# A ring of four PSUM banks for the first eight steps of the last layer, and products nobody reads in TensorE's wait before it

## The reference

```python
x = _attn_ref(q, k, v)                      # 2 x 8 heads, 576 tokens, top 32 scores kept
x = _moe_ref(x, w_gate, w1, w2, capacity)   # 1152 tokens, 8 experts of 288 slots, relu
# the last layer, 1152 tokens, 512 -> 2048 -> 512
h = x @ w_in
h2 = h * h
h3 = h2 * h
P = a[0] + a[1] * h + a[2] * h2 + a[3] * h3
Q = 1.0 + np.abs(b[0]) * np.abs(h) + np.abs(b[1]) * h2
g = P / (Q + 1e-06)
return (g @ w_out).astype(np.float32)
```

## Time and profile before

| | |
|---|---|
| median of 3 runs | 807.46 us |
| lowest, highest | 806.16, 808.84 us |
| the profiled execution | 809.16 us |
| its span (first to last instruction) | 807.4 us |
| mean granted TensorE clock over the span | 0.958 |

### The profile page before, as it was taken

The page is one execution under the profiler, slowest core; times in us unless marked ns, Lnnn a source line. Parts: engine busy times, 40 slices in busy tenths (PEclk is TensorE's granted clock), DMA queues, the critical chain, the costliest instruction groups (busy, mean ns, idle before and its releaser), DMA issues.

```text
span 807.4 us, 15534 instructions
## 1 busy us (share of the span) xinstructions
PE 740.2 (92%) x5370; PEld 692.8 (86%) x5370; DVE 658.3 (82%) x1664; ACT 491.8 (61%) x890; POOL 359.7 (45%) x531
## 2 busy tenths in 40 slices
PE   4899999999999999838999999999469999999997
PEld 4788899898898888728999999999469899898996
DVE  3999999999999999825767667675749988898885
ACT  6677676666677775434445444544547767767673
POOL 4646565545568784240000000000149678667764
PEclk9799999999999999967999999999769999999999
DMA  9640000600000202031657677586811002000001
GB/s 190 159 163 14 1 16 1 222 15 2 14 2 15 106 7 100 1 144 44 219 173 237 194 207 238 170 210 190 230 48 31 1 1 80 1 0 19 22 1 39
DMA packets 61978, 71.20 MB, mean 88 GB/s; under 512 B 21969, under 2 KB 41937, under 8 KB 61906
## 3 DMA queue, kind: packets, MB, share of 16 engines
q1 hardware_dynamic: 60466, 65.57, 27.5%
q0 software_dynamic: 1440, 4.72, 1.7%
HBM read 56.12 MB, written 14.16 MB: 87 GB/s over the span
## 4 chain that ended last, share of the span: by engine, by line
PE 58%; DVE 26%; DMA 5%; issue 4%; ACT 3%; POOL 2%; SPq 1%; DVEq 0%; ACTq 0%; POOLq 0%
PE bank L1400 16%; PE bank L1401 16%; PE bank L1402 16%; DVE best L739 8%; DVE pairs L741 5%; DVE best L760 3%; PE bank L1306 3%; DVE pairs L758 2%; PE bank L1282 2%; PE bank L1272 2%; DMA slots_out<-y_blocks 2%; DVE pairs L722 2%; DMA slot_rows<-slots_in 2%; DVE joined L769 1%; DVE least_kept L778 1%
## 5 line engine op out<-in xcount | busy, mean ns | idle before, releaser
L957 DVE RECIPROCAL r<-c 128x384 f32<-128x384 f32 x48 | 122.5, 2552 | 25.3 <-POOL c L678 25.2
L739 DVE MAX8 best<-pairs 128x8 f32<-128x288 f32 x288 | 130.9, 547 | 0.0
L1028 ACT ACTIVATE probsT<-bank 96x768 f32<-96x768 f32 x72 | 58.2, 808 | 95.5 <-PE bank L1289 95.5
L667 POOL DMA_INDIRECT x_rows<-slots_out,slot_index x9 | 11.2, 1240 | 225.8 <-DMA slots_out<-y_blocks 224.3
L1306 PE MATMUL bank<-v_rows,probsT 96*128 96x65 f32 (+1 forms) x960 | 106.5, 264 | 3.6 <-ACT probsT L1028 3.4
L741 DVE MATCH_REPLACE8 pairs<-best,pairs 128x288 f32<-128x288 f32 x216 | 109.7, 547 | 0.0
L1306 PEld LDWEIGHTS bank<-v_rows,probsT 96*128 96x128 f32 (+1 forms) x960 | 102.3, 181 | 8.0 <-ACT probsT L1028 6.8
L886 DVE TENSOR_TENSOR wl<-raw,wh 128x1024 fp32r<-128x1024 f32 x72 | 87.2, 1218 | 19.6 <-ACT wh L1122 19.2
L1136 ACT ACTIVATE hTh<-bank 128x288 fp32r<-128x288 f32 x64 | 26.5, 414 | 104.4 <-PE bank L1402 104.4
L1400 PE MATMUL bank<-xTh,wh 128*128 128x288 f32 x256 | 76.7, 300 | 12.9 <-DVE xTl L898 12.9
L577 POOL TENSOR_TENSOR pairs<-scores 128x288 int32<-128x288 int32 x72 | 57.7, 801 | 66.3 <-ACT scores L1014 65.9
(11 more groups left out here) (138 smaller groups left out, 2201.6 us busy)
## 6 DMA issues: line engine op xcount, KB each, us to landing
raw<-in_moe_w SPq DMA_DIRECT2D x16, 2048.0 KB, 8.9
slots_in<-zeros SPq DMA_DIRECT2D x18, 256.0 KB
slot_rows<-slots_in SPq DMA_DIRECT2D x32, 144.0 KB, 8.7
slots_out<-y_blocks SPq DMA_DIRECT2D x32, 144.0 KB, 8.2
raw<-in_moe_w_in SPq DMA_DIRECT2D x8, 512.0 KB, 8.0
v_rows<-in_v SPq DMA_DIRECT2D x16, 144.0 KB, 4.0
out_rows<-out_rows SPq DMA_DIRECT2D x9, 256.0 KB, 2.4
q_rows<-in_q SPq DMA_DIRECT2D x8, 256.0 KB, 3.1
```

Source lines behind the costliest of these rows:

```text
L739: ins = nc.vector.max(best, cur)
L957: nc.vector.reciprocal(rS[x][:], cS[x][:]).then_inc(s_d2, 1)
L1028: nc.scalar.activation(pT[x % 2][:], T_ps[0:KP, 0:KJ * P], ACT.Exp, scale=SCALE).then_inc(s_ex, 1)
```

## The change

It has three parts.

1. PE issues 38 matmuls of 128x512 into bank 0 after the last expert product, from weights that are ready by then, and three more after each of the three tiles' transposes. Nobody reads what they write: `in_step(0)` starts bank 0 afresh.
2. The first eight steps' hidden values lie in banks 0, 1, 2, 6, 0, 1, 2, 7 in place of 0, 1, 2, 0, 1, 2, 0, 1. Steps 3 and 7 wait for no g, steps 4 to 6 wait for g of steps 0 to 2 (four steps back), steps 8 to 10 for g of steps 4 to 6, and from step 11 on all is as before, three steps back.
3. Since banks 6 and 7 are lent to steps 3 and 7, the transposes for the next group come after steps 10 to 13, for both groups that have them, on PE, ACT and DVE alike.

```diff
-        T_AT = (8, 9, 10, 11)
+        T_AT = (10, 11, 12, 13)
+        H2_FIRST = (0, 1, 2, 6, 0, 1, 2, 7)
+        def h2_bank(m):
+            return bank(H2_FIRST[m] if m < len(H2_FIRST) else (m - len(H2_FIRST)) % 3)
+        def h2_steps_before(m):
+            return 0 if m in (0, 1, 2, 3, 7) else m - 3 if m < 11 else m - 2
...
-                hp = bank(m % 3)[:, 0:GN]
+                hp = h2_bank(m)[:, 0:GN]
...
+            def keep_busy(times, to, by):
+                for _ in range(times):
+                    nc.tensor.matmul(to, by[:, 0:P], by[:, 0:to.shape[1]], start=True, stop=True)
...
             w2_step(E - 1, 1, FC - 1)
             pe.wait_ge(s_yt, E * DC)
+            pe.wait_ge(s_wl, 4 * (2 * E - 1))
+            keep_busy(38, bank(0), wh[0])
...
                         if i == TG - 1:
                             last.then_inc(s_tb[t_use(d)[0]], 1)
+                    keep_busy(3, bank(0), wh[0])
...
             def in_step(m):
                 g, f = divmod(m, FC2)
-                if m >= 3:
-                    pe.wait_ge(s_g, m - 2)
+                if h2_steps_before(m):
+                    pe.wait_ge(s_g, h2_steps_before(m))
...
-                    last = product(bank(m % 3)[:, 0:GN], wh[sl][:, c:c + P], wl[sl][:, c:c + P],
+                    last = product(h2_bank(m)[:, 0:GN], wh[sl][:, c:c + P], wl[sl][:, c:c + P],
```

## The result

| | before | changed |
|---|---|---|
| median of 4 timed runs, us | 808.04 | 801.75 |
| lowest, highest, us | 806.16, 808.84 | 801.33, 802.91 |
| profiled execution, us (its span) | 809.16 (807.4) | 802.91 (801.2) |
| mean granted TensorE clock | 0.958 | 0.972 |

The ratio is 0.9929 with a 95% interval from 0.9912 to 0.9947, so 5.7 us faster (4.3 to 7.1); the two medians lie 6.3 us apart. It was forecast as 4.6 us, with a median of 802.9.

The account below looks back on a forecast made before the run. PE was taken as the bound from out(0) on, so an earlier out(0) counts in full: 5.2 us less 0.3 gives 4.9, 4.6 against the median, forecasting 802.9 us, range 800.9 to 805.8.

Parts of the forecast that it names:

- step 0: Step after the gathers: held by the tokens' low parts, it lets step 1 start at 595.3, not 596.54; 1.25 us.
- steps 1 and 2: Next two steps on PE: their first matmuls, low before, now run at the high clock; 0.35 us gained.
- the wait: PE's 2.21 us wait for g before step 3 shrinks to 0.3 us before step 4; 1.9 us gained.
- steps 3 and 4: The two steps ahead of out(0): at the high clock 4.18 us in place of 5.90; 1.7 us gained.
- The ties at out(1) and out(2): PE gets to these two outs about when gl(1) and gl(2) end; 0.3 us charged.
- Part 1, the fillers: Gather wait and tiles: 38 matmuls, 10 low, end at 587.6; clock back before step 0 is half done.
- Rival (b): The clock isn't held over the gathers, so step 0 runs low; 3.8 to 2.1 us gained, 804.6; chance 0.16.
- Part 2, the ring: Steps 0 to 3 run without a wait, step 4 waits 0.3 us; out(0) at 604.0, 5.2 us earlier.
- Part 3, the turns: The same eight turns of three transposes, two steps later: nothing added, 3 us of cover left before step 16.
- (c): DVE's chain sets the pace, gl late at steps 5 and 6 and their outs; 2 to 3 us gained, 805.2; chance 0.09.
- (d): The wait at step 4 grows and the clock falls there; 1 to 2 us gained, 806; chance 0.05.
- (e): Slower: fillers run low throughout, end at 593.4, and step 0 starts 8 us later; 811; chance 0.04.

Follow-up runs that it names:

- Ring alone: The changed kernel without any of the 47 filler matmuls; 31.26 us to out(0) against 35.20 before, timed gain 4.3 us (2.8 to 5.7).
- fillers alone: The kernel before plus the 47 filler matmuls, banks and transposes as before; 33.52 us to out(0), timed gain 1.2 us (0.3 to 2.1).
- 60 fillers: The changed kernel with 60 matmuls in the wait in place of 38; 33.68 us to out(0), timed gain 3.2 us (2.1 to 4.4).
- turns alone: The kernel before with only the next group's transposes moved to steps 10 to 13; 35.30 us to out(0), ratio 0.9992 (0.9977 to 1.0006).
- one lent bank: The changed kernel with bank 6 lent to step 3 only, bank 7 taken back; 29.88 us to out(0), timed gain 1.5 us (0.5 to 2.5).

## Why the prediction was right

**The measure.** PE is the bound from out(0) on and the change only shifts it: right, 193.73 and 193.74 us.

**The size.** 5.2 us to out(0) less 0.3 for late gl was forecast, 5.14 measured. By terms: step 0 gave 1.37 (forecast 1.25), steps 1 and 2 0.37 (0.35), the wait 1.93 (1.9), steps 3 and 4 1.47 (1.7), since they took 4.43 us without the wait where I had 4.18. The ties at out(1) and out(2) cost nothing: gl(1) ended at 606.95 and out(1) started at 607.09, gl(2) at 611.12 and out(2) at 611.31. I then took off 0.3 more because the timed median of before lay under the profiled execution and I ascribed part of it to low clock. That step was wrong, though the clock does have a part in the spread: all timed executions of the kernel before, beside the experiments, with a mean clock of 0.958 to 0.961 took 807.3 to 810.0 us, those at 0.963 to 0.966 took 804.9 to 807.1. But in the profiles that difference lies far ahead of the change. Between 20 and 60 us the mean clock was 0.89 to 0.91 in the six that came first to the scattering of the tokens (345.1 to 345.7 us) and 0.87 in the four that came last (347.6 to 347.8), whose programs are the same up to there. So it touches nothing that the change gains, and nothing was to be taken off. The stretch up to out(0) varied by up to 0.24 us between profiles of like kernels, the part ahead of the change by 2.7. By the timed ratio the gain is 5.7, which does not exclude 5.1.

**Part 1, the fillers.** The 38 ran from 575.68 to 585.95, low for 2.87 us and 7 of them, where I had 4.3 us and 10. Step 1 came 1.37 us earlier (21.19 against 22.56 from the last expert matmul), forecast 1.25. But the prediction let the 38 carry the clock and the threes only keep it, and there the right number came with a wrong share. The runs showed that the threes with their transposes raise it by themselves in time for step 0, and that the 38 are worth 0.25 to 0.36 us beside them by the spacing of the tiles (0 to 0.5 at out(0)) and nothing without them. Rival (b), that it isn't held over the gathers, is what happens with the 38 alone, and costs 1.4 us (31.42 against 30.06).

**Part 2, the ring.** The wait at step 4 was 0.28 us, forecast 0.3; step 3 ran at the high level. Ring alone shows 3.9 us, the whole wait of 2.21 and the 1.7 of steps 3 and 4: without the wait the fall behind it goes too.

**Part 3, the turns.** No cost, shown by a run of its own (35.30 against 35.20).

**The other rivals.** (c) showed only with one bank lent or three in the ring: then DVE's chain does set the pace, at step 7 or step 4. (d) did not occur; nearest to it is the fillers alone, where the cost moved on by a step. (e) was shown as a mechanism by the 60 fillers.

## What to carry to other kernels

When a stage starts with a pipeline of several engines behind it, count how many steps the first engine can issue before the first result comes back and give the ring that many buffers for those steps only, from banks that the steady state uses later; it must last until the slower chain has caught up. Work that nobody reads paid here just ahead of the real work, between the last landings (1.2 us for 9 matmuls), and hardly in the long wait before them (0 to 0.5 us for 38); so test the parts alone. And measure a small change inside the program, from the last common instruction to the first point behind which all is equal, where the whole time spreads by more than the effect.

## What the hardware showed that I had not expected

- Transposes of 128x128 in fp32 raise the granted clock: 45 of them, back to back, from 0.50 to 1.00 within 3.6 us.
- The clock came back within 3.1 us when PE had four transposes and three 128x512 matmuls a tile at the low level, while in the kernel before, with the transposes alone and 2 us of gaps, it was still 0.50 four microseconds into step 0.
- Idle times of nearly the same length had either outcome: behind 2.21 us (before), 2.35 (turns alone) and 2.31 us (one lent bank) the clock fell within 0.5 us of the next matmul, behind 2.36 us and then 1.21 (fillers alone) it did not.
- Two executions of the same instructions on the same inputs reached the end of the experts up to 2.7 us apart, nearly all of it in the attention, and the latest four had the lower clock between 20 and 60 us (0.87, against 0.89 to 0.91 in the earliest six). What sets that clock was not looked for.
